# Attention and two expert layers on one core: scores of two key tiles as one product, sinks' values ahead of the last values, first weight sums two rounds later

## What is computed

```python
scores = q @ k.transpose(0, 1, 3, 2) / sqrt(64)         # B=2, H=8, S=768, D=64
keep = (key < 4) | ((0 <= query - key) & (query - key < 128))
a = exp(where(keep, scores, -1e9) - max);  a = a / (a.sum(-1) + 1e-9)
x = (a @ v) as 1536 tokens x 512
p = domain_probs / (domain_probs.sum(-1) + 1e-9)         # 4 experts
y = sum over e of p[:, e] * (relu(x @ w1[e]) @ w2[e])     # 512 -> 1024 -> 512
h = y @ w_in;  out = (h * cos(h)) @ w_out                # 512 -> 2048 -> 512
```

## Time and profile before

| | |
|---|---|
| three runs | 863.51, 863.89, 864.95 us (median 863.89) |
| the profiled execution | 860.06 us |
| its span, first to last instruction | 858.3 us |
| TensorE's granted clock, mean | 0.996 of full speed |
| attention rounds | 0 to about 101 us of the span |
| TensorE, weight loads, VectorE, ScalarE, GpSimd busy | 98%, 87%, 54%, 53%, 63% |

### The profile page before, as it was taken

How to read it: one execution, slowest core, us unless ns; L and a number is a source line. 1 busy time by engine, 2 the same in 40 slices (tenths; PEclk the granted TensorE clock), 3 DMA queues, 4 the chain that set the end, 5 groups by cost and what they waited for, 6 DMA issues and landing times.

```text
span 858.3 us, 13943 instructions
## 1 busy us (share of the span) xinstructions
PE 842.5 (98%) x4756; PEld 751.0 (87%) x4756; DVE 461.1 (54%) x952; ACT 458.7 (53%) x984; POOL 541.1 (63%) x408
## 2 busy tenths in 40 slices
PE   8899899999999999999999999999999999899998
PEld 6788789989988988988988998998898998898997
DVE  6678633433433427533433433348757759747756
ACT  6587734334334336423423423526867869767864
POOL 3699776556466775675475475867385396584450
PEclk9999999999999999999999999999999999999999
DMA  9794331211311220321131121120220230530201
GB/s 168 175 204 114 98 99 50 99 50 50 99 52 48 98 72 27 99 99 35 65 99 39 60 99 50 50 99 26 73 99 19 81 99 1 173 99 3 96 0 74
DMA packets 73156, 67.31 MB, mean 78 GB/s; under 512 B 40608, under 2 KB 46848, under 8 KB 73088
## 3 DMA queue, kind: packets, MB, share of 16 engines
q1 hardware_dynamic: 73088, 66.42, 26.0%
HBM read 62.96 MB, written 3.19 MB: 77 GB/s over the span
## 4 chain that ended last, share of the span: by engine, by line
PE 90%; issue 3%; DVE 2%; POOL 1%; ACT 1%; DMA 1%; SPq 1%; ACTq 0%; POOLq 0%
PE scores L1278 11%; PE scores L1282 10%; PE scores L1280 10%; PE scores L1308 10%; PE scores L1310 10%; PE scores L1306 10%; PE bank L1308 5%; PE bank L1310 5%; PE bank L1306 5%; PE bank L1278 3%; PE bank L1282 3%; PE bank L1280 3%; PE bank L1224 2%; PE scores L1187 1%; DVE x_lo L952 1%
## 5 line engine op out<-in xcount | busy, mean ns | idle before, releaser
L555 POOL TENSOR_TENSOR w_lo<-w_raw,w_hi 128x512 fp32r<-128x512 f32 x96 | 128.6, 1349 | 184.3 <-ACT w_hi L669 184.3
L1278 PE MATMUL scores<-x_hi,w_hi 128*128 128x384 f32 x528 | 178.6, 338 | 4.0 <-ACT kept L701 2.6
L1282 PE MATMUL scores<-x_hi,w_lo 128*128 128x384 f32 x528 | 177.3, 336 | 0.0
L1280 PE MATMUL scores<-x_lo,w_hi 128*128 128x384 f32 x528 | 177.3, 336 | 0.0
L562 POOL TENSOR_TENSOR w_lo<-w_raw,w_hi 128x1024 fp32r<-128x1024 f32 x48 | 116.8, 2444 | 65.6 <-ACT w_hi L679 65.6
L679 ACT ACTIVATE w_hi<-w_raw 128x1024 fp32r<-128x1024 f32 x48 | 50.7, 1059 | 189.7 <-PE scores L1310 189.7
L1308 PE MATMUL scores<-w_lo,h_hi 128*128 128x512 f32 x384 | 149.7, 390 | 0.0
L1310 PE MATMUL scores<-w_hi,h_lo 128*128 128x512 f32 x384 | 149.7, 390 | 0.0
L1306 PE MATMUL scores<-w_hi,h_hi 128*128 128x512 f32 x384 | 149.4, 389 | 0.0
L1278 PEld LDWEIGHTS scores<-x_hi,w_hi 128*128 128x128 f32 x528 | 99.6, 189 | 6.4 <-issue 5.6
L1050 DVE SCALAR_TENSOR_TENSOR acc<-scores,probs,acc 128x512 f32<-128x512 f32 x56 | 41.8, 749 | 116.3 <-PE scores L1310 116.3
(11 more groups left out here) (126 smaller groups left out, 1582.4 us busy)
## 6 DMA issues: line engine op xcount, KB each, us to landing
w_raw<-in_moe_w_dram SPq DMA_DIRECT2D x32, 1024.0 KB, 5.1
w_raw<-in_moe_w_in_dram SPq DMA_DIRECT2D x8, 1024.0 KB, 5.0
w_raw<-in_moe_w_out_dram SPq DMA_DIRECT2D x8, 1024.0 KB, 5.1
v_nat<-in_v_dram SPq DMA_DIRECT2D x12, 256.0 KB, 3.5
norm<-routing_dram SPq DMA_DIRECT2D x24, 128.0 KB, 3.2
out_dram<-acc SPq DMA_DIRECT2D x12, 256.0 KB, 4.2
k_nat<-in_k_dram SPq DMA_DIRECT2D x11, 256.0 KB, 4.8
q_nat<-in_q_dram SPq DMA_DIRECT2D x11, 256.0 KB, 5.2
```

The costliest lines, as they stand in the source:

```text
L555: nc.gpsimd.tensor_tensor(w1_slots(w1_lo, h % 2, part), w1_part(h % 2, part), w1_slots(w1_hi, h % 2, part).bitcast(F32), ALU.subtract)\
L1278: nc.tensor.matmul(target[:, 0:HALF], w1_hi[:, i, slot, d], x_hi[:, n - 1, d], start=first and d == 0, stop=False, skip_group_check=True)
L1280: nc.tensor.matmul(target[:, 0:HALF], w1_hi[:, i, slot, d], x_lo[:, n - 1, d], start=False, stop=False, skip_group_check=True)
L1282: last = nc.tensor.matmul(target[:, 0:HALF], w1_lo[:, i, slot, d], x_hi[:, n - 1, d], start=False, stop=d == 1, skip_group_check=True)
```

## The change

1. `k_t` is laid out with the pairs outermost, and `scores` of a tile that is not the first of a sequence multiplies two whole slots, its own and that of the tile ahead, 264 columns in the order of the slots, as one product for each head. Where the own part lies is told by `own_at`. The sink columns of slot 0 are set to zero once, since the first tile of a sequence has none.
2. In even rounds `weigh_sinks` comes ahead of `weigh_values`; ScalarE's `copy_out` waits for the two in the other order.
3. `sum_weights(0, ...)`, `first_lo`, `first_hi` of the first weight block come two rounds later, `sum_tokens(0, ...)` one round later.
4. `tokens_hi` waits only for the sum that it reads, or for the tiles themselves where it reads no sum.
5. Some tiles of SBUF lie at other places.

```diff
+        def own_at(t):
+
+            return SLOT if later(t) and t % 3 else 0
+
+        def prev_at(t):
+
+            return SLOT - own_at(t)
...
             made_one(nc.gpsimd.memset(quarter[:], QUARTER))
+            made_one(nc.gpsimd.memset(k_t[:, :, 0, P:SLOT], 0.0))
...
-                if 5 <= i < 9:
-                    sum_weights(0, i - 5)
-                if 10 <= i < 16:
-                    first_lo(*divmod(i - 10, 3))
+                if 7 <= i < 11:
+                    sum_weights(0, i - 7)
+                if 12 <= i < 18:
+                    first_lo(*divmod(i - 12, 3))
                 if i % 2 == 0 and 0 <= (i - 6) // 2 < T:
                     normalise((i - 6) // 2)
-                if 17 <= i < 21:
-                    sum_tokens(0, i - 17)
+                if 18 <= i < 22:
+                    sum_tokens(0, i - 18)
...
             def copy_out(t):
-                act.wait_ge(pv_done, 2 * (t + 1))
                 if later(t):
                     act.wait_ge(sinks_done, sinks_before(t + 1))
+                act.wait_ge(pv_done, 2 * (t + 1))
...
                 n = PRODUCTS[i]
-                act.wait_ge(x_summed, 4 * (b + 1))
+                if n in (7, 5, 6, 4):
+                    act.wait_ge(x_summed, 4 * b + (7, 5, 6, 4).index(n) + 1)
+                elif b < 2:
+                    act.wait_ge(x_ready, TPB * (b + 1))
+                else:
+                    act.wait_ge(x2_ready, TPB * (b - 1))
...
-                if 9 <= i < 15:
-                    first_hi(*divmod(i - 9, 3))
+                if 11 <= i < 17:
+                    first_hi(*divmod(i - 11, 3))
...
-                    nc.vector.copy_predicated(score_banks[j % 2][:, :, 0:P],
+                    nc.vector.copy_predicated(score_banks[j % 2][:, :, own_at(t):own_at(t) + P],
                                               in_prev[:].bitcast(mybir.dt.int32).unsqueeze(1).broadcast_to([P, 2, P]),
-                                              score_banks[j % 2][:, :, PREV:PREV + P]).then_inc(merged, 1)
+                                              score_banks[j % 2][:, :, prev_at(t):prev_at(t) + P]).then_inc(merged, 1)
...
-                parts = [(t % 3, width(t), 0)]
-                if later(t):
-                    parts.insert(0, ((t - 1) % 3, P, PREV))
-                for slot, cols, at in parts:
-                    for r in range(2):
-                        rows = slice(r * D, (r + 1) * D)
-                        last = nc.tensor.matmul(score_banks[j % 2][:, r, at:at + cols],
-                                                q_t[rows, t % 2, p, :], k_t[rows, slot, p, 0:cols],
-                                                start=True, stop=True)
+                for r in range(2):
+                    rows = slice(r * D, (r + 1) * D)
+                    if later(t):
+                        low, high = sorted((t % 3, (t - 1) % 3))
+                        keys = k_t[rows, p, low:high + 1:high - low, :]
+                        target = score_banks[j % 2][:, r, 0:2 * SLOT].rearrange("q (n k) -> q n k", n=2)
+                    else:
+                        keys = k_t[rows, p, t % 3, 0:P]
+                        target = score_banks[j % 2][:, r, 0:P]
+                    last = nc.tensor.matmul(target, q_t[rows, t % 2, p, :], keys, start=True, stop=True)
                 last.then_inc(scores_done, 1)
...
                 if 0 <= n < ND:
-                    weigh_values(n)
                     if n % 2 == 1 and later(n // 2):
                         weigh_sinks(n // 2)
+                    weigh_values(n)
```

More of the change, by code:

```diff
@@ L51, in program @@
     WIN = P + SINK
-    PREV = 2 * P
     SLOT = P + SINK
@@ L127, in program @@
         v_nat = sb("v_nat", [P, 3, DM], stack=att)
+        weights_t = sb("weights_t", [P, SLOTS, 2, 4, P], stack=att)
         weights = sb("weights", [P, 2, H, WIN], stack=att)
-        weights_t = sb("weights_t", [P, SLOTS, 2, 4, P], stack=att)
         sink_w = sb("sink_w", [P, 2, 3, HS], F32R, stack=att)
@@ L132, in program @@
         v_sink = sb("v_sink", [3 * HS, B, DM], F32R, stack=att)
+        q_t = sb("q_t", [P, 2, PAIRS, P], stack=att)
         neg_max = sb("neg_max", [P, T, H], stack=att)
@@ L139, in program @@
         masked = sb("masked", [P, AHEAD, WIN], stack=att)
-        k_t = sb("k_t", [P, 3, PAIRS, SLOT], stack=att)
+        k_t = sb("k_t", [P, PAIRS, 3, SLOT], stack=att)
         k_sink = sb("k_sink", [P, PAIRS, SINK], stack=att)
-        q_t = sb("q_t", [P, 2, PAIRS, P], stack=att)
         q_nat = sb("q_nat", [P, 2, DM], stack=att)
@@ L507, in sink_keys @@
                         pool.wait_ge(k_sink_ready, sinks_before(t))
-                    nc.gpsimd.tensor_copy(k_sink[:], k_t[:, t % 3, :, 0:SINK]).then_inc(k_sink_kept, 1)
+                    nc.gpsimd.tensor_copy(k_sink[:], k_t[:, :, t % 3, 0:SINK]).then_inc(k_sink_kept, 1)
                 else:
@@ L512, in sink_keys @@
                         pool.wait_ge(scores_done, PAIRS * (t - 1))
-                    nc.gpsimd.tensor_copy(k_t[:, t % 3, :, P:SLOT], k_sink[:]).then_inc(k_sink_ready, 1)
+                    nc.gpsimd.tensor_copy(k_t[:, :, t % 3, P:SLOT], k_sink[:]).then_inc(k_sink_ready, 1)
             def lower_values(b):
@@ L752, in gated_hi @@
                 nc.scalar.activation(h_part(h_hi, h % 2, c), c_source(h % 2, c), ACT.Copy).then_inc(hi_ready[c], 1)
-            copy_half(turn_bank, 0, k_t[:, 0, 0:2, 0:P], (first_turned, 1), first_ready)
+            copy_half(turn_bank, 0, k_t[:, 0:2, 0, 0:P], (first_turned, 1), first_ready)
             copy_half(out_bank, 0, q_t[:, 0, 0:2], (first_turned, 2), first_ready)
-            copy_half(weights_bank, 2, k_t[:, 0, 2:4, 0:P], (k_turned, 1), first_ready)
+            copy_half(weights_bank, 2, k_t[:, 2:4, 0, 0:P], (k_turned, 1), first_ready)
             copy_half(sums_bank, 2, q_t[:, 0, 2:4], (q_turned, 1), first_ready)
@@ L894, in mask_head @@
                 nc.vector.tensor_tensor_reduce(
-                    out=masked[:, n % AHEAD, 0:width(t)], in0=score_banks[j % 2][:, r, 0:width(t)], in1=m[:],
+                    out=masked[:, n % AHEAD, 0:width(t)], in0=score_banks[j % 2][:, r, own_at(t):own_at(t) + width(t)], in1=m[:],
                     scale=-(float(D) ** -0.5), scalar=3.0e38, op0=ALU.add, op1=ALU.min,
@@ L904, in copy_keys @@
                     dve.wait_ge(k_sink_kept, (t - 3) // TPB + 1)
-                nc.vector.tensor_copy(k_t[:, t % 3, :, 0:P], turn_bank[:].rearrange("p (k s) -> p k s", k=PAIRS))\
+                nc.vector.tensor_copy(k_t[:, :, t % 3, 0:P], turn_bank[:].rearrange("p (k s) -> p k s", k=PAIRS))\
                     .then_inc(k_ready, 1)
```

## The result

The changed kernel takes 857.65 us (median of 4 runs, 857.01 to 858.90) where the kernel before takes 863.83 (4 runs, 863.51 to 864.95): ratio 0.9928, 95% interval 0.9911 to 0.9945. A second comparison, of 8 and 23 runs, gave 858.16 beside 862.07: 0.9948 (0.9924 to 0.9973). So it is 4 to 6 us faster, by more than a measurement is uncertain; 859.6 (857.2 to 862.4) was forecast. The profiled executions show less: 860.06 before, 857.01 after, spans 858.3 and 855.2, a gain of 3.05 us where 4.35 were forecast for them. Where the other microseconds are is the first question for the experiments.

The account below looks back on a forecast made before the run. TensorE, 98% busy, was taken to bound the kernel, with GpSimd as full in the attention part. Turning round 24 at 85.95 instead of 90.30 gains 4.35 us: 860.06 becomes 855.7 profiled, 859.6 for the median; range 857.2 to 862.4.

Parts of the forecast that it names:

- Part 1: Rounds 7 and 8: weight sums two rounds later end TensorE's wait for sink gathering and half clock; gain 4.26 us.
- the gain carries over: Whole kernel: the 4.35 us gained on the profiled execution also comes off the runs' median of 863.89, giving 859.6.
- GpSimd's queue: Attention rounds: GpSimd becomes late, so TensorE waits 0.5, 0.4 and 2.1 us for gatherings in rounds 11, 21 and 23.
- The contention: Gathering of round 22: VectorE's x_lo beside the token sum costs GpSimd 0.72 us; by the skill's rule 1.08.
- Part 2: ScalarE's x_hi copies wait for less, so TensorE's pauses of 1.04 and 0.89 us in front of L1200 go.
- From there to the end nothing changes: After round 24's turning at 85.95 instead of 90.30 nothing more is gained or lost; gain 4.35 us.
- TensorE's side alone: Rival that GpSimd is no hindrance: round 24 at 82.9, gain 7.4 us, total 856.5; chance 0.12.
- the rival in which GpSimd takes most of it back: GpSimd's norm wait stays 1.84 us, round 23's pause grows to 3.9, clock costs 1.7; gain 0.8, 863.1; chance 0.17.
- The forecast's line of 2.47 us: TensorE's pause in round 7, after which the clock fell; a longer pause in round 23 would cost 1.7 us again.
- part 3: Score bursts: 4 products of 264 columns replace 8; columns set the pace, a 0.3 us loss hidden by GpSimd's lateness.
- part 4: Even rounds: sinks ahead of the last values are the same products in another order, with inputs a round old; 0.
- The slower rival: Score bursts: row halves no longer run beside each other, up to 2.2 us a burst; about 878 us; chance 0.05.

Follow-up runs that it names:

- experiment 1: The kernel before, unchanged, profiled once more (the second profile before): ratio 0.9998, profiled 862.59 us.
- the five profiles with the old sums: Kernel before, profiled twice, and before with only ScalarE's shorter waits, only the merged product, or only the new order of sinks and values; rounds 7 and 8: 9.53 to 14.10 us.
- two variants with the old sums: Kernel before with only ScalarE's shorter waits, 1.0012, and with only the merged product, 1.0005.
- the six profiles with the later sums and the old order of transfers and gatherings: Changed kernel twice (second 858.16 us); it with old sink order, 0.9945, or last token sum later, 0.9964; before with later sums, 0.9979, plus ScalarE's shorter waits, 0.9948.
- Experiments 3 to 5: Kernel before with the later sums alone, 0.9979; with ScalarE's shorter waits alone, 1.0012; with both, 0.9948.
- experiment 2: The changed kernel, unedited, run and profiled again (the second profile after): 858.16 us beside 862.07 for the kernel before.
- the order alone: Kernel before with the sinks' values ahead of the last values and nothing else: 0.9995.

## Why the prediction was right, and where not

**The number was near partly by luck.** 859.6 was forecast and 857.65 measured, close to the fast end of the range; the second comparison has 858.16. The sum was made for the profiled execution, and there 3.05 us came instead of 4.35. The medians gained 6.2 and 3.9 us; most likely the timed runs of before met later transfers and more half clock than its first profile (experiment 1). So one miss made up for the other. Two slips in the working are small: 84.6 less 82.4 is 2.2 us of wait and not 2.1 (3.1 in all), and 863.89 less 4.35 is 859.5.

**Part 1 was right, and its size a draw.** Rounds 7 and 8 gained 4.47 us; 4.26 was summed. Against the second profile before they gain 5.46, against the five profiles with the old sums 2.6 to 7.2. The step "the gain carries over" to the median has no ground for that reason: the pauses end with a transfer whose landing varied, and the half clock behind the first lasted 3.4 us in both profiles before, 6.8 in two variants with the old sums, and stayed away in a third. Whether 4.35 was too small for the medians stays open: 6.2 in one comparison, 3.9 in the other. The later sums take TensorE's dependence on w_raw away. What is left is GpSimd's wait for norm, and it varies too (its first product began at 29.94 to 31.39 us in the six profiles with the later sums and the old order of transfers and gatherings), but TensorE's wait in round 11 was only 0.23 to 0.86 us in them.

**GpSimd's queue was right.** Forecast: first x_t product 30.8, gatherings done at 43.2, 76.2 and 84.6. Measured: 30.80; done at 43.16, about 76.0 and 84.39. That 30.8 is met exactly is luck, as the second profile has 29.94; the gatherings of rounds 20 and 22 were done at 75.98 and 84.35 there all the same. Waits forecast 0.5, 0.4 and 2.1 us, measured 0.86, 0.92 and 2.19. From round 9 to 23 a loss of 0.25 was summed (0.65 less 0.9) and 0.21 came out, but with two terms missing that cancel: waits longer by 0.9, and six even rounds shorter by 0.2 each. Round 24 is turned at 86.59, 0.6 us behind the forecast of 85.95, because of the half clock; without it, in the second profile, at 85.85.

**The contention was right in size.** While VectorE's L966 ran from 80.39, GpSimd's L489 took 1.35 us instead of 0.63: 0.72 more, as taken from the earlier trace rows, on the parting and not on the sum. By the Trainium skill ("SBUF — State Buffer", Who interferes with whom) the later of the two stands until the other is done. The prediction took VectorE's full length for that, 1.08 us. What is left of VectorE's instruction when GpSimd's begins is the better reading: 0.86 us here, 0.84 for L538 at 85.54, which lost 0.70. Read so, the rule and the rows agree to 0.15 us.

**Part 2 was mis-stated.** It was summed as a gain of its own. Experiments 3 to 5 show it as the condition of part 1: nothing alone, and without it the later sums lose behind round 23 (8.64 us, half clock included, instead of 5.28 to 5.99) most of what they gain in rounds 7 and 8. The sum got the total nearly right since it took both.

**"From there to the end nothing changes" was wrong.** From the turning of round 24 to the product the changed kernel took 0.85 us more in one profile and 2.16 in the other. In the first it is the half clock, which ran until 88.5 us, 1.9 us past the turning, and so cost about 1 us (an estimate: half of 1.9). In the second it is a wait of 2.38 us for the last gathering. GpSimd's queue was followed to the gathering of round 22 and no further. Between that one and the last stand three instructions that VectorE's L966 stretched (L538, L489, L500, 0.7 us each, 2.14 in all), where before had only one lengthened by 0.06 (L477 at 89.54) and one of 0.74 in the last gathering itself (L494 at 91.09), for which TensorE did not wait. GpSimd and, last row, VectorE of before:

```profile
87.66 1.27 POOL L529 TENSOR_TENSOR x_t<-x_t,norm 128x512 f32<-128x512 f32 x1
...
91.09 0.99 POOL L494 TENSOR_TENSOR sink_w<-weights,sink_w 128x32 fp32r<-128x32 f32 x1
...
88.37 1.37 DVE L952 TENSOR_TENSOR x_lo<-x_t,x_hi 128x768 fp32r<-128x768 f32 x1
```

Of the 7.4 us that TensorE's side alone would have gained, this and the waits before it are what is not there.

**The clock of the rival in which GpSimd takes most of it back** came without that rival's norm wait of 1.84 us (none in the first profile, 0.81 at 45.51 in the second): a half clock after 2.19 us of pause in one profile, none after 2.18 in the other. The forecast's line of 2.47 us was not one. Where it fell, the product came no later, as a wait swallowed it; of the time forecast for that rival (863.1) nothing came.

**Parts 3 and 4**: 0 in the time within the intervals, as summed. For part 3 the reason holds, a burst of 1.16 us. For part 4 the step "the same products in another order, 0" is wrong on TensorE, where it is 0.2 us in an even round, and right in the total. The slower rival, halves that no longer run side by side, is out with the burst's 1.16 us.

## What to carry to other kernels

Where one profiled execution is shorter than the timed runs, look which pauses end with a transfer: their length is a draw, and a change that takes the dependence away gains their mean, not what the profile happened to show. A second profile of the kernel before, or the mean clock of its timed runs, tells. Follow a queue that has become the pacemaker to its last waiter, not to the last one that waited before. And look for the wait that a moved step stretches on a third engine: a producer moved later loses much of its worth (here about half) until its other consumers stop waiting for all of it.

## What the runs showed of the hardware

- The half clock is not settled by a kernel: after pauses of 2.18 and 2.19 us at the same place one execution had it and one had not. Over the 14 profiles, ahead of the first product of w_hi with x_hi into a bank, it lasted 3.413 us in eight, 6.827 in four and stayed away in two. By the mean clocks of the 31 runs in experiment 1, each 3.413 us of it goes with some 1.8 us of time (3.6 us between the means at 0.994 and at 0.998); where a wait follows that can swallow it, as in experiment 2, it costs nothing.
- Two of TensorE's products start 0.11 us apart within a shape, but 0.20 at each change between scores (64 rows), transposes, and values of 64 weight columns, and between values and sinks (96 rows). Only from transposes to sinks, both of 128 weight columns, the distance is 0.03. An even round of before has four changes of 0.20; with the sinks between transposes and values, in the order alone as in the changed kernel, it has three and the short one, and that is 0.17 of the 0.2 us. Whether it is the weight load that nothing covers there was not tried.
- Four products of 264 columns take what eight of 128 or 132 took, 1.16 and 1.17 us: at these widths columns, not instructions, set the pace of two half-array products side by side.
- A VectorE subtraction of 128x768 that had begun up to 0.4 us ahead of a GpSimd instruction stretched that one by 0.7 us, whether it was a cast of 0.24 us, a selection of 0.63 or a product of 1.27. Where GpSimd's had begun first it kept its length (L529 of before, 1.27 us at 87.66), and VectorE's was the one that took longer (L952 at 88.37, 1.37 us instead of 1.08).
